# An opening program of its own for the first three chunks of a fused attention and two-expert kernel

## The chip, the cores and the metric

The kernel runs on one core of one Trainium2 chip. The metric is the device time of a whole execution in microseconds (us); lower is better. The kernel before took 826.4 us in the median of 3 runs (826.23 to 827.62).

The engines are named as in the profile: PE is TensorE (PEld its loading of weights), DVE is VectorE, ACT is ScalarE, POOL is GpSimd, SP is SyncE, which only issues transfers.

## The reference

```python
# attention with a decayed state: 4 batches, 8 heads, 768 tokens, 48 channels
for t in range(S):
    cur = einsum('bhd,bhe->bhde', u[None] * k[t], v[t])
    y[t] = einsum('bhd,bhde->bhe', r[t], state + cur)
    state = w[t][:, :, :, None] * state + einsum('bhd,bhe->bhde', k[t], v[t])
x = y.transpose(0, 2, 1, 3).reshape(3072, 384)
# first expert: 384 -> 1024 -> 384
h = x @ w_in
e = exp(h - max(h)); solu = h * e / (sum(e) + 1e-9)
ln = (solu - mean(solu)) / sqrt(var(solu) + 1e-6) * g_ln
x2 = ln @ w_out
# second expert: 384 -> 2048 -> 384
h2 = x2 @ w_in2
out = maximum(0.01 * h2, h2) @ w_out2
```

All arrays are float32.

## The kernel before, in words

**Tiles.** The 768 tokens of a batch are 6 chunks of 128 tokens. Three chunks are one super-tile of 384 tokens, so that there are 24 chunks and 8 super-tiles. Heads go in 4 pairs. TensorE has two ways to multiply: a float32 product, which the trace shows as two instructions, and an fp32r product of one instruction. Every large matrix product is made of three fp32r products: both operands are split into a high part (a copy that is rounded to fp32r) and a low part (the value less the high part), and high by high, low by high and high by low are added up. So each of the four weight matrices (W1 and W2 of the first expert, W3 and W4 of the second) stands in SBUF as `W1H`, `W1L` and so on. The raw load of a matrix lies where its low part will be (`W1raw` over `W1L`).

**A chunk is 8 items.** Item s=1 transposes the chunk's end keys (`transpose_keys`), s=2 to 5 make the scores of the 4 pairs (TensorE, masked by VectorE in `mask`), s=3 to 6 multiply the masked scores by the values and the queries by the state (`attend` in the changed kernel), s=6 also makes the fresh state, s=7 transposes y and splits it, and s=8 is the product by W1 (`expert_in`, 18 instructions with 512 columns). Softmax and layer norm of the 1024 hidden values follow in the next chunk's items: `row_max`, `exp_rows`, `times_exp`, `row_stats`, `row_moments`, `row_scale` (GpSimd), `normalise`. `prepare` makes the decays of the next chunk: four scans, four reciprocals, one product (VectorE), then `decayed_queries` and `end_keys` on GpSimd.

**A super-tile is 24 steps.** 8 steps M1 transpose the normalised rows (`prod`, three transposes), split them and multiply them by W2 (`cons`, nine instructions with 384 columns). 16 steps M2 multiply by W3 (`prod`, nine instructions), take the leaky maximum, split and multiply by W4 (`cons`, nine). `cons` runs two steps behind `prod`. Beside every step one item of a coming chunk is issued, on every engine in the order of the program text. The items lead by `LEAD` = 28: before the first M1 step items 1 to 28 are run alone (chunks 0 to 2, and half of chunk 3), and when the first M2 step begins 36 items are done.

**The weights.** ScalarE makes the high parts and VectorE or GpSimd the low parts, in 18 pieces of 1024 columns, tied to items by the table `when`. W2 is first multiplied by the layer norm's gain on GpSimd (L471). TensorE waits for all of W1's pieces before the first chunk's second half of columns, for W2's before the first M1 step and for W3's and W4's before the first M2 step (`wait_split`). SyncE loads chunk m+2's decays and chunk m+1's tokens when chunk m's buffers come free: there are two buffers of `att` and one of the tokens.

## Time and profile before

| | us |
|---|---|
| median of 3 runs | 826.4 |
| the profiled execution's own time | 825.48 |
| its span | 823.7 |
| first M2 product starts (from the span's start) | 114.25 |
| TensorE busy in the span | 786.2 (95%) |
| VectorE busy | 521.3 (63%) |
| GpSimd busy | 196.7 (24%) |

The page's slices cut the span into 40 parts of 20.6 us, each digit being the busy share in tenths. A row of a group gives line, engine, operation, output and inputs, shape and count, then busy time in us and mean ns of one, then the idle time of the engine ahead of it with what ended it. A time of the timeline is counted from the span's start; a row there can be several like instructions merged, and its duration holds the pipeline's delay, so that what an instruction costs is read from the start of one to the start of the next. The windows give the same busy times for stretches that one chooses.

### The profile page before, as it was taken

To read this page: it belongs to the slowest core of one execution; us is meant where nothing else is said; L and a number is where in the kernel's file an instruction comes from. 1 tells how busy PE (TensorE), PEld (TensorE's weight loads), DVE (VectorE), ACT (ScalarE), POOL (GpSimd) and SP (SyncE) were. 2 spreads that over 40 slices of the span, in tenths; PEclk is the share of its full clock that TensorE was granted. 3 is DMA by queue.
4 is the path that set the end of the run, shared out by engine and by line. 5 is a ranking of instruction groups with operands and counts; after the bars stand their busy time and mean duration, and the time that the engine had idled before them with its cause. 6 is when DMAs were issued, how large, how long until landed. Compare 5 with 4: busy or idle time off the path is not lost.

```text
span 823.7 us, 11957 instructions
## 1 busy us (share of the span) xinstructions
PE 786.2 (95%) x4570; PEld 746.2 (91%) x4570; DVE 521.3 (63%) x1068; ACT 338.8 (41%) x652; POOL 196.7 (24%) x216
## 2 busy tenths in 40 slices
PE   2877999999999999999999999999999999999996
PEld 2655999999999999999999999999999999999996
DVE  7778776576575676667665765666765775553332
ACT  3335644344433444434434444335443444334332
POOL 4477823113111221121221131122131121000000
PEclk9976899999999999999999999999999999999999
DMA  7772211203202302203202122113112030000000
GB/s 193 248 228 58 58 30 29 58 2 87 58 1 58 87 1 58 58 1 88 58 1 58 28 61 58 29 29 87 29 30 58 1 87 30 1 1 29 1 0 32
DMA packets 18847, 43.50 MB, mean 53 GB/s; under 512 B 2272, under 2 KB 14688, under 8 KB 18400
## 3 DMA queue, kind: packets, MB, share of 16 engines
q1 hardware_dynamic: 14736, 33.24, 16.5%
q10 hardware_dynamic: 4048, 9.44, 3.3%
q8 instruction: 37, 0.61, 0.3%
q14 instruction: 26, 0.21, 0.1%
HBM read 37.95 MB, written 4.72 MB: 52 GB/s over the span
## 4 chain that ended last, share of the span: by engine, by line
PE 85%; DVE 0%; ACT 0%; issue 0%; ACTq 0%
PE BANKS L964 60%; PE MISC L964 21%; PE BANKS L1075 2%; PE MISC L994 1%; PE MISC L987 1%; DVE Rraw L863 0%; DVE RL L869 0%; ACT RH L633 0%; ACT Rraw L626 0%; DVE X2L L875 0%; ACT X2H L638 0%; ACT OUT L644 0%; DVE A L745 0%; DVE nmean L817 0%; ACTq L248 0%
## 5 line engine op out<-in xcount | busy, mean ns | idle before, releaser
L626 ACT ACTIVATE Rraw<-BANKS 128x384 f32<-128x384 f32 x128 | 62.9, 492 | 239.5 <-PE BANKS L964 237.8
L863 DVE TENSOR_TENSOR Rraw<-BANKS,Rraw 128x384 f32<-128x384 f32 x128 | 71.3, 557 | 133.5 <-ACT Rraw L626 133.0
L964 PE MATMUL BANKS<-RH,W4H 128*128 128x384 f32 x384 | 138.6, 361 | 0.9 <-DVE RL L869 0.8
L964 PE MATMUL BANKS<-X2H,W3H 128*128 128x384 f32 x384 | 130.4, 339 | 0.2 <-DVE X2L L875 0.2
L964 PE MATMUL BANKS<-X2L,W3H 128*128 128x384 f32 x384 | 129.1, 336 | 0.0
L964 PE MATMUL BANKS<-RL,W4H 128*128 128x384 f32 x384 | 129.1, 336 | 0.0
L964 PE MATMUL BANKS<-X2H,W3L 128*128 128x384 f32 x384 | 129.0, 336 | 0.0
L964 PE MATMUL BANKS<-RH,W4L 128*128 128x384 f32 x384 | 129.0, 336 | 0.0
L633 ACT ACTIVATE RH<-Rraw 128x384 fp32r<-128x384 f32 x128 | 67.1, 524 | 73.2 <-DVE Rraw L863 73.2
L436 POOL TENSOR_TENSOR ke<-att 112x512 f32<-112x512 f32 x24 | 29.5, 1230 | 255.3 <-DVE att L739 255.3
L735 DVE RECIPROCAL ki<-att 112x128 f32<-112x128 f32 x96 | 90.1, 941 | 0.0
L869 DVE TENSOR_TENSOR RL<-Rraw,RH 128x384 fp32r<-128x384 f32 x128 | 72.5, 567 | 23.1 <-ACT RH L633 23.1
L460 POOL TENSOR_TENSOR rstd<-vare,mhalf 128x1 f32<-128x1 f32 x24 | 18.5, 771 | 245.2 <-DVE vare L818 245.2
L964 PE MATMUL MISC<-rb,att 112*128 112x256 f32 x192 | 61.3, 403 | 13.9 <-DVE att L739 13.3
L964 PEld LDWEIGHTS BANKS<-RH,W4H 128*128 128x128 f32 x384 | 72.3, 188 | 2.4 <-DVE RL L869 1.4
L964 PEld LDWEIGHTS BANKS<-RH,W4L 128*128 128x128 f32 x384 | 72.5, 189 | 1.0
L964 PEld LDWEIGHTS BANKS<-X2H,W3H 128*128 128x128 f32 x384 | 72.1, 188 | 0.5 <-issue 0.5
L964 PEld LDWEIGHTS BANKS<-X2H,W3L 128*128 128x128 f32 x384 | 72.1, 188 | 0.0
L964 PEld LDWEIGHTS BANKS<-RL,W4H 128*128 128x128 f32 x384 | 72.1, 188 | 0.0
L964 PEld LDWEIGHTS BANKS<-X2L,W3H 128*128 128x128 f32 x384 | 72.1, 188 | 0.0
L964 PE MATMUL BANKS<-RH,W2H 128*128 128x384 f32 x192 | 68.8, 358 | 0.0
L964 PE MATMUL BANKS<-RL,W2H 128*128 128x384 f32 x192 | 64.7, 337 | 0.0
(117 smaller groups left out, 1509.3 us busy)
## 6 DMA issues: line engine op xcount, KB each, us to landing
att<-rkw SPq DMA_DIRECT2D x48, 288.0 KB, 4.9
rtok<-r_tok SPq DMA_DIRECT2D x24, 192.0 KB, 4.5
ktok<-k_tok SPq DMA_DIRECT2D x24, 192.0 KB, 4.6
vtok<-v_tok SPq DMA_DIRECT2D x24, 192.0 KB, 4.7
out<-OUT SPq DMA_DIRECT2D x8, 576.0 KB, 5.6
W3raw<-w_in ACTq DMA_DIRECT2D x1, 3072.0 KB, 11.2
W4raw<-w_out ACTq DMA_DIRECT2D x1, 3072.0 KB, 24.3
W1raw<-w_in ACTq DMA_DIRECT2D x1, 1536.0 KB, 9.5
```

The lines of the kernel that those rows point to most:

```text
L436: nc.gpsimd.tensor_tensor(ke[:, :, :], kt[:, p, :, :], last, ALU.mult).then_inc(pool_ke, 1)
L460: nc.gpsimd.tensor_tensor(rstd[:, :], vare[:, :], mhalf[:, :], ALU.pow).then_inc(pool_rstd, 1)
L626: nc.scalar.activation(Rraw[:, fp % 2, :], PR[fp % 2][:, 0:ST], ACT.Copy, scale=0.01).then_inc(act_slope, 1)
L633: nc.scalar.activation(RH[:, fp % 2, :], src, ACT.Copy).then_inc(act_hi, 1)
L735: nc.vector.reciprocal(ki[:, a, :], ct[:, m % 2, a, :]).then_inc(dve_inv, 1)
L863: nc.vector.tensor_tensor(Rraw[:, fp % 2, :], PR[fp % 2][:, 0:ST], Rraw[:, fp % 2, :], ALU.max).then_inc(dve_relu, 1)
L869: nc.vector.tensor_tensor(RL[:, fp % 2, :], full, RH[:, fp % 2, :].bitcast(F32), ALU.subtract).then_inc(dve_lo, 1)
L964: return nc.tensor.matmul(dst, lhsT, rhs, start=start, stop=stop, skip_group_check=True)
L987: last = nc.tensor.transpose(XT[:, k * CH:(k + 1) * CH], rtok[:, k * 128:(k + 1) * 128], ident[:, :])
L994: last = nc.tensor.transpose(keys_of(b, m)[:, a * PD:(a + 1) * PD], ke[:, a, :], ident[0:PD, 0:PD])
L1075: last = nc.tensor.transpose(dst[:, c * CH:(c + 1) * CH], LN[:, c, f * 128:(f + 1) * 128], ident[:, :])
```

## The change

The first three chunks no longer go through items and M1 steps. They have an order of their own, written out for each engine.

- Decays, keys, queries and tokens of chunks 0, 1 and 2 have a buffer each (`att2`, `tok12`, `A2` lie in the space of W4's high part, which is filled later), and SyncE issues all their loads at the start. ScalarE issues the loads of W1, W3 and W2 one behind the other.
- For these chunks both products of the first expert are float32 products on the raw weights: `first_expert` is 6 products with 512 columns (two instructions each) in place of 18 fp32r ones, and `first_out` is 24 products with 128 columns for each chunk. y and the normalised rows are not split. The rows are transposed by `first_rows` and multiplied by the gain on the way out of PSUM (`take_ln`, 8 ACTIVATEs of 128 columns).
- W1 and W2 are split later, in the first M2 steps, and W2's gain is no longer multiplied in by GpSimd; later M1 steps multiply by it when they take the rows from PSUM (ScalarE and VectorE, `step` and `step_lo`).
- All low parts are made by GpSimd (`low_part`), in 24 groups of 768 columns: W3's eight and W4's first while the opening runs, the other 15 in the 16 steps of the first M2 stage.
- The opening ends with 24 items done (chunks 0 to 2). The first M2 stage has 28 items in its 16 steps in place of 16, so that from the first M1 step on the items stand as before.
- In the opening the scans read their floor from PSUM (`FLOOR_PS`), masks are made for two pairs at once, and the first chunk's keys in two halves.
- TensorE multiplies the identity by itself eight times, unread, before the first scores.

```diff
+        if opening and fp <= STEPS:
+            done = [CPS * SLOTS + (F1 + LEAD - CPS * SLOTS + F2) * j // F2 for j in (f, f + 1)]
+        else:
+            done = [fp + LEAD - 1, fp + LEAD]
+        listed.append((k, so, f, fp, [slot_of(i) for i in range(done[0] + 1, done[1] + 1)]))
...
+        att2 = sb("att2", [PD, 3, PAIRS, CH], over="W4H", skip=3 * F2 * MODEL // 8 * 4)
+        A2 = sb("A2", [CH, PAIRS, 2, CH], over="W4H")
...
+        tok12 = [sb(f"tok{m}", [CH, 3, MODEL], over="W4H", skip=(5 * F2 // 8 + 3 * (m - 1)) * MODEL * 4) for m in (1, 2)]
...
+        FLOOR_PS = PR[1][0:PD, 511:512]
...
-        when = {0: 3, 1: 5, 2: 7, 3: 15, 4: 16, 5: 17, 6: 18, 7: 20, 8: 21, 9: 23, 10: 23, 11: 23,
-                12: 27, 13: 28, 14: 29, 15: 30, 16: 31, 17: 32}
-        by_dve = (0, 1, 2, 3, 4, 9, 10, 11)
...
+        GROUPS = (4, 4, 8, 8)
...
-            load_T(0, 1)
-            for i in range(1, LEAD + 1):
-                item(0, *slot_of(i))
-            for kind, so, f, fp, m, s in first_steps():
-                item(0, m, s)
+            for m in (1, 2):
+                load_T(0, m)
+                load_tok(0, m)
+            load_tok(0, 3)
+            load_T(0, 4)
+            load_T(0, 3)
...
+            def low_part(w, g):
+                pool.wait_ge(split_hi[w], g + 1)
+                if w == 0:
+                    pool.wait_ge(pe_h, 2 * CPS)
+                if w == 1:
+                    pool.wait_ge(pe_cons, F1)
+                nc.gpsimd.tensor_tensor(group(los[w], w, g), group(raws[w], w, g),
+                                        group(his[w], w, g).bitcast(F32), ALU.subtract).then_inc(split_lo[w], 1)
...
+                    if opening(b, kind, so):
+                        if f % 2 == 0 and f // 2 + 1 < GROUPS[3]:
+                            low_part(3, f // 2 + 1)
+                        if f < GROUPS[0]:
+                            low_part(0, f)
+                        if F1 <= f < F1 + GROUPS[1]:
+                            low_part(1, f - F1)
...
+            decayed_queries(0, 2)
+            decayed_state(0, 1)
+            own_token(0, 1, 1)
+            own_token(0, 2, 0)
+            end_keys(0, 2)
+            decayed_state(0, 2)
+            own_token(0, 2, 1)
+            row_scale(0, 0)
+            for g in range(2):
+                low_part(2, g)
+            row_scale(0, 1)
+            for g in range(2, 4):
+                low_part(2, g)
+            row_scale(0, 2)
+            decayed_queries(0, 3)
+            for g in range(4, 6):
+                low_part(2, g)
+            end_keys(0, 3)
+            for g in range(6, 8):
+                low_part(2, g)
+            low_part(3, 0)
...
+            take_keys(0, 0)
+            part_heads(0, 1)
+            take_x(0, 0)
+            take_range(0, 1)
+            take_keys(0, 1)
+            part_heads(0, 2)
+            take_range(0, 2)
+            take_x(0, 1)
+            take_keys(0, 2)
+            load_weights(3)
+            exp_rows(0, 0)
+            for g in range(2):
+                high_part(2, g)
+            take_x(0, 2)
+            normalise(0, 0)
+            exp_rows(0, 1)
+            take_ln(0)
+            normalise(0, 1)
+            exp_rows(0, 2)
+            for g in range(2, 4):
+                high_part(2, g)
+            take_ln(1)
+            normalise(0, 2)
+            for g in range(4, 6):
+                high_part(2, g)
+            part_heads(0, 3)
+            for g in range(6, 8):
+                high_part(2, g)
+            take_ln(2)
+            take_range(0, 3)
+            for g in range(2):
+                high_part(3, g)
+            take_x2(0, 0)
+            for g in range(4):
+                high_part(0, g)
...
+                    nc.scalar.activation(RH[:, fp % 2, :], PR[fp % 2][:, 0:ST], ACT.Identity,
+                                         scale=gain[:, f:f + 1]).then_inc(act_hi, 1)
...
+            decay(0, 1)
+            first_mask(0, 0)
+            own_sums(0, 0)
+            first_mask(0, 2)
+            for a in (0, 1):
+                inverse(0, 1, a)
+            take_y(0, 0)
+            take_state(0, 0)
+            for a in (2, 3):
+                inverse(0, 1, a)
+            undecayed_keys(0, 1)
+            decay(0, 2)
+            for a in (0, 1):
+                inverse(0, 2, a)
+            for a in (0, 2):
+                first_mask(1, a)
+            own_sums(0, 1)
+            for a in (2, 3):
+                inverse(0, 2, a)
+            undecayed_keys(0, 2)
+            take_y(0, 1)
+            take_state(0, 1)
+            for a in (0, 2):
+                first_mask(2, a)
+            own_sums(0, 2)
+            row_max(0, 0)
+            take_y(0, 2)
+            take_state(0, 2)
+            times_exp(0, 0)
+            row_stats(0, 0)
+            row_moments(0, 0)
+            row_max(0, 1)
+            times_exp(0, 1)
+            row_stats(0, 1)
+            row_moments(0, 1)
+            row_max(0, 2)
+            times_exp(0, 2)
+            row_stats(0, 2)
+            row_moments(0, 2)
+            decay(0, 3)
+            for a in range(PAIRS):
+                inverse(0, 3, a)
+            undecayed_keys(0, 3)
+            take_x2(0, 0)
...
+            def first_expert(m, halves=(0, 1)):
+
+                pe.wait_ge(act_x, m + 1)
+                if m == 0:
+                    pe.wait_ge(ld_w[0], 16)
+                if m == 1:
+                    pe.wait_ge(dve_masked, CPS * PAIRS)
+                for n in halves:
+                    for k in range(KM):
+                        last = mm(hidden(0, m)[:, n * 512:(n + 1) * 512], X[:, k, :], w1[:, k, n * 512:(n + 1) * 512],
+                                  k == 0, k == KM - 1)
+                    last.then_inc(pe_h, 1)
...
+            def first_rows(m):
+
+                pe.wait_ge(act_ln, m + 1)
+                if m == 0:
+                    pe.wait_ge(dve_decay, CPS * PAIRS)
+                    pe.wait_ge(dve_state, CPS)
+                if m == 1:
+                    pe.wait_ge(dve_he, 4)
+                for f in range(F1):
+                    if m == 2 and f % 4 == 0:
+                        pe.wait_ge(act_lnT, F1 + f + 4)
+                    last = nc.tensor.transpose(ln_bank(m, f // 4)[:, f % 4 * CH:(f % 4 + 1) * CH],
+                                               LN[:, m, f * 128:(f + 1) * 128], ident[:, :])
+                    if f % 4 == 3:
+                        last.then_inc(pe_lnT, 1)
...
+            def first_out(m):
+
+                if m == 0:
+                    pe.wait_ge(dve_he, 4)
+                    pe.wait_ge(ld_w[1], 16)
+                for f in range(F1):
+                    pe.wait_ge(act_lnT, m * F1 + f + 1)
+                    for k in range(KM):
+                        last = mm(ACC[k][:, m * CH:(m + 1) * CH], w2[:, f, k * 128:(k + 1) * 128], first_ln[:, f, :],
+                                  m == 0 and f == 0, f == F1 - 1)
...
+            for _ in range(8):
+                mm(ACC[0][:, 0:128], ident[:, :], ident[:, :], True, True)
+            first_scores(0, range(PAIRS))
+            first_attend(0, (0, 1))
+            first_keys(0)
+            first_attend(0, (2, 3))
+            first_state(0)
+            first_transposes(0)
+            first_expert(0, (0,))
+            first_scores(1, range(PAIRS))
+            first_keys(1)
+            first_attend(1, range(PAIRS))
+            first_state(1)
+            first_scores(2, range(PAIRS))
+            first_expert(0, (1,))
+            first_transposes(1)
+            first_keys(2)
+            first_attend(2, range(PAIRS))
+            first_state(2)
+            first_expert(1)
+            first_transposes(2)
+            first_rows(0)
+            first_expert(2)
+            first_out(0)
+            for m in (1, 2):
+                first_rows(m)
+                first_out(m)
             for b in range(B - 1):
-                run(b, batch_steps(False))
+                run(b, batch_steps(False, b == 0))
```

The order on TensorE at the start of the first M2 stage, before (`RH`, `RL` are split rows, `X2H`, `X2L` the split input of the second expert, `rb` and `att` the operands of scores, `A` the masked scores, `vtok` the values):

```order
238 L964 MATMUL BANKS<-RH,W2L 128x384
239 L964 MATMUL BANKS<-RL,W2H 128x384
240 L964 MATMUL MISC<-rb,att 128x256 [waits dve_masked,split_lo2,split_lo]
241 L964 MATMUL MISC<-state,att 128x96 [waits dve_masked]
242 L964 MATMUL MISC<-vtok,A 128x48 x2
243 L964 MATMUL BANKS<-X2H,W3H 128x384 [waits dve_x2,dve_lo]
```

The same place after (`OUT` holds the transposed rows, `W2raw` the raw weights, `ke` the end keys):

```order
110 L1122 MATMUL BANKS<-OUT,W2raw 128x128 [waits act_lnT]
111 L1122 MATMUL BANKS<-OUT,W2raw 128x128 x2
112 L1122 MATMUL BANKS<-OUT,W2raw 128x128 [waits act_lnT]
113 L1122 MATMUL BANKS<-OUT,W2raw 128x128 x2
114 L1146 MATMUL MISC<-ident,ke 128x112 [waits pool_ke,dve_state]
115 L1146 MATMUL MISC<-ident,ke 128x112 x3
116 L1122 MATMUL BANKS<-X2H,W3H 128x384 [waits dve_x2,split_lo2]
```

The item ahead of the first M2 product is now item 25 (chunk 3, s=1) and was item 37 (chunk 4, s=5).

The order on GpSimd from the second chunk's queries to the end of the opening, after (`tok_84` are chunk 2's tokens, `att_74` its decays, queries and keys; `W3L` is a low part):

```order
37 L502 TENSOR_TENSOR tok_84<-tok_84,diag 128x384 [waits dve_diag]
38 L510 TENSOR_TENSOR rstd<-vare,mhalf 128x1 [waits dve_var]
39 L512 TENSOR_TENSOR nbias<-nmean,rstd 128x1 [waits pool_rstd]
40 L520 TENSOR_TENSOR W3L<-W3raw,W3H 128x3x256 [waits split_hi2] x2
41 L510 TENSOR_TENSOR rstd<-vare,mhalf 128x1 [waits act_ln,dve_var]
42 L512 TENSOR_TENSOR nbias<-nmean,rstd 128x1 [waits pool_rstd]
43 L520 TENSOR_TENSOR W3L<-W3raw,W3H 128x3x256 [waits split_hi2] x2
44 L510 TENSOR_TENSOR rstd<-vare,mhalf 128x1 [waits act_ln,dve_var]
```

Low parts of W3 now stand between the row scales of the three chunks, where the queue of before had pieces of W2 and W3.

## Rows read from the trace of the kernel before

**Rows 1.** The page: busy time, then TensorE and its granted clock in 40 slices.

```profile
PE 786.2 (95%) x4570; PEld 746.2 (91%) x4570; DVE 521.3 (63%) x1068; ACT 338.8 (41%) x652; POOL 196.7 (24%) x216
...
PE   2877999999999999999999999999999999999996
...
PEclk9976899999999999999999999999999999999999
```

**Rows 2.** Windows, all engines: stretch, length, busy by engine (instructions), granted clock, DMA.

```profile
27.00:113.23 86.23, 71.97 (x332) 60.84 (x332) 66.01 (x128) 41.38 (x66) 61.70 (x50) 0.80 0.44 128
113.23:182.47 69.24, 69.23 (x411) 66.65 (x410) 44.99 (x95) 28.25 (x57) 12.31 (x14) 1.00 0.14 35
182.47:207.73 25.26, 25.26 (x155) 23.89 (x156) 17.31 (x37) 11.78 (x24) 6.63 (x8) 1.00 0.27 71
```

**Rows 3.** The chain that ended last: start, us, what (merged).

```profile
117.67 1.43 PE MISC L964 x14
...
124.14 4.19 PE MISC L964 x18
...
765.13 47.95 PE BANKS L964 x270
```

**Rows 4.** Timeline of TensorE: start, duration, instruction, count.

```profile
27.58 0.63 PE L964 MATMUL BANKS<-W1L,XH 128*128 128x512 f32 x1
...
28.01 0.63 PE L964 MATMUL BANKS<-W1H,XL 128*128 128x512 f32 x1
...
92.42 0.49 PE L1075 MATMUL BANKS<-ident,LN 128*128 128x128 f32 x3
92.70 0.50 PE L964 MATMUL MISC<-W1H,XH 128*128 128x512 f32 x1
...
113.23 0.60 PE L964 MATMUL MISC<-rb,att 112*128 112x256 f32 x2
113.66 0.35 PE L964 MATMUL MISC<-state,att 112*128 112x96 f32 x2
113.86 0.57 PE L964 MATMUL MISC<-vtok,A 128*128 128x48 f32 x4
114.25 0.42 PE L964 MATMUL BANKS<-X2H,W3H 128*128 128x384 f32 x1
```

**Rows 5.** Windows, TensorE alone: stretch, length, busy, granted clock, DMA.

```profile
28.00:29.00 1.00, 1.00 (x4) 1.00 0.85 154
...
57.00:66.00 9.00, 8.94 (x39) 0.50 0.00 0
90.00:91.00 1.00, 1.00 (x8) 0.76 0.00 0
```

**Rows 6.** Timelines of VectorE and GpSimd, in this order.

```profile
7.84 1.37 DVE L727 TENSOR_TENSOR_SCAN att<-att,floor 112x128 f32<-112x128 f32 x4 [3.56 <-DMA att<-rkw]
...
13.81 3.28 DVE L727 TENSOR_TENSOR_SCAN att<-att,floor 112x128 f32<-112x128 f32 x4 [0.59 <-DMA att<-rkw]
...
92.56 3.13 DVE L739 TENSOR_TENSOR att<-att,ki 112x512 f32<-112x512 f32 x1
...
88.06 7.08 POOL L477 TENSOR_TENSOR W4L<-W4raw,W4H 128x1024 fp32r<-128x1024 f32 x3
```

**Rows 7.** Groups by form: VectorE (first two), ScalarE (two), GpSimd (one).

```profile
L735 DVE RECIPROCAL ki<-att 112x128 f32<-112x128 f32 x96 | 90.1, 941 | 0.0
...
L798 DVE TENSOR_TENSOR LN<-MISC,LN 128x512 f32<-128x512 f32 x28 | 18.0, 687 | 7.5 <-ACT LN L560 7.5
...
L567 ACT ACTIVATE LN<-EXP,nbias,rstd 128x1024 f32<-128x1024 f32 x8 | 9.9, 1243 | 3.9 <-POOL nbias L462 3.5
...
L555 ACT ACTIVATE W4H<-W4raw 128x1024 fp32r<-128x1024 f32 x6 | 6.2, 1048 | 0.0
...
L428 POOL TENSOR_TENSOR att<-att 112x508 f32<-112x508 f32 x24 | 30.7, 1281 | 7.1 <-DVE att L727 7.1
```

**Rows 8.** DMA issues of the first 60 us: size, median us to landing.

```profile
ub<-u SPq DMA_DIRECT2D x1, 192.0 KB, 6.2
```

More of the change, by code:

```diff
@@ L61, in slot_of, with batch_steps @@
     return (item - 1) // SLOTS, (item - 1) % SLOTS + 1
-def batch_steps(last):
+def batch_steps(last, opening=False):
     out = []
@@ L1008, in item @@
                 p = m % 2
-                if first(b, m) and 1 <= m and 1 <= s <= 3:
-                    expert_in(b, m - 1, s - 1, 3)
-                if s == 1 and not first(b, m):
+                if s == 1:
                     if m % CPB > 0:
```

541 lines of the change are left out of this document (291 added, 250 removed).

## The prediction

> **What bounds the kernel now.** I read the page first. TensorE is busy 95% of the span, and all that is missing lies in the first five slices and the last; the granted clock is below full only there too [rows 1]. The windows then cut the start by stage [rows 2]. From 113.23 us on TensorE has no gap: 69.23 of 69.24 us in the first M2 stage, 25.26 of 25.26 in the next M1 stage. From 27 to 113.23 it is busy 71.97 of 86.23 us at a mean clock of 0.80. So behind the first M2 product, which starts at 114.25 [rows 4], the kernel costs what TensorE has to do, and ahead of it what chains between engines and the low clock allow. The end is the start of that product plus a fixed remainder, 823.7 - 114.25 = 709.45 us. The change earns what it brings that start forward, and pays for the items that it then has still to run.
>
> **Prices on TensorE at full clock.** Starts in a row give them [rows 4]: a pair's scores 0.43 us (two instructions of 256 columns), its state product 0.20, its values 0.39 (four instructions of 48 columns), three transposes 0.28. An fp32r `expert_in` is 4.19 us, and the 14 instructions of item 6 are 1.43, so the fresh state is 1.43 - 0.59 = 0.84 [rows 3]. A float32 product has two instructions of 0.215 us per 256 columns. That makes 0.86 us for 512 columns and 5.2 us for a `first_expert`, and 0.215 us for 128 columns, 5.2 us for a `first_out`. At low clock both double, as 512 columns of fp32r do: 0.43 us from start to start at 28 us [rows 4], and 4.19/18 = 0.23 at full clock [rows 3]. The granted clock of that window reads 1.00 [rows 5], so before the first change of clock I go by the spacing, which is 1.2 GHz.
>
> **The opening, step by step.** DVE: first scans 1.37 us [rows 6], a reciprocal 0.94 (0.84 from start to start), a product of 512 columns 0.69 [rows 7], and I take a maximum or a statistics instruction of that width alike. ACT: normalise 1.24, high parts of 768 columns 1.05 x 0.75 = 0.8 [rows 7], the exponent, as wide as the normalise, 1.3; an ACTIVATE of 128 columns 0.27 by estimate, an eighth of 1.05 and as much again for its start. POOL: queries 1.28 [rows 7], low parts 7.08/3 x 0.75 = 1.8 [rows 6].
> - Chunk 0. The decays land at about 7.4 (0.4 earlier, fewer memsets ahead of the load). POOL now waits for `ub` before its first queries: `ub` took 6.2 us to land [rows 8], which is about 10.8. First scores follow at 12.4, behind ScalarE's copies. The scores at low clock take 3.4 us, masks, values, keys and fresh state run to 22.2, y is transposed by 23.1 and the first expert starts at 23.8 (before: 27). The eight products of the identity run from about 5 to 8.4 us, where TensorE has nothing else; cost 0.
> - First half of expert 0 at low clock 5.1 us, to 28.9. Scores of chunk 1 (keys ready at 25.4) follow, then masks and values, state, scores of chunk 2 at 35, the second half of expert 0 to 39.4, values of chunk 2 from 40.2 to 43.8.
> - Expert 1 from 43.8: the small products ahead of it leave the clock low. Of its 5.2 us some 2.3 double: to 51.5. y of chunk 2 at 52; ACT takes it (0.5) and only then normalises chunk 0 (1.24): rows at 53.7, TensorE waits 1.8 us. Transposes 0.8, expert 2 5.2: 59.7. Out 0: 65. Rows and out 1: 71.1. Rows 2 at 71.9. ACT has in its order by then one normalise, 6 high parts and the queries of chunk 3, 1.24 + 4.8 + 1.3 behind 66+2.2, so that `take_ln(2)` starts at about 73.8; out 2 to 79.4, X2 split, first M2 product at 81. Before: 114.25.
>
> From both sides: with no wait after 23.8 and full clock, three experts and three outs (31 us), two chunks' attention and the rest (14 us) end at 69. With the low clock for all that is not expert or out, and 4 us more of waits, at 89. I take 81, from the chain.
>
> **What it pays.** 12 items are moved behind that point: chunk 3 without its first and chunk 4's s=1 to 5. A whole chunk by these prices is 4.19 + 0.28 + 0.4 + 4 x (0.43 + 0.59) + 0.84 = 9.8 us, by the windows (69.24 - 16 x 18 x 47.95/270)/2 = 9.05 [rows 2, 3]; I take 9.5. Chunk 3 less its keys' transposes is 9.1, chunk 4's five 0.4 + 4 x 0.43 + 3 x 0.59 = 3.9: together 13.0 us.
>
> The first M2 stage becomes 69.2 + 13 = 82.3 us for TensorE. VectorE had 44.99 us in it with two chunks of items [rows 2]; 16 steps are about 18 of these, so a chunk is 13.5 and 3.5 chunks 47: 65 of 82. POOL gets 3.5 x 6.2 + 15 x 1.8 = 49. Cover is there, but items now stand two to a step. From the end of an expert to the scores that may overwrite its sums, maximum, exponent and product need 0.7 + 0.2 + 1.3 + 1.3 + hops, 4.1 us, and TensorE has about 3.6 us of work between them, where it had two whole steps: some 1 to 1.5 us lost for each of three chunks. ScalarE also does four high parts of W1 (3.2 us) ahead of the first M2 step, about 1 us. I take 5 us; the ends are 0 and 14. The gain moved into M1's copies costs nothing: VectorE is busy 17.31 of 25.26 us there and TensorE has no gap [rows 2], and GpSimd is rid of its eight products. The loads carry the bytes of before and stand earlier in their queues. Two matrices and two chunks more are now in flight at once, but W1 is wanted at 23.8 and chunk 1's tokens at 31; I take 0, and if the tokens came a few us late it would lie in the 89 above, no further.
>
> The last item is the port. The product of keys took 3.13 us, where one of the same width takes 0.69 [rows 7], while POOL made three low parts in a row [rows 6]; scans took 3.28 instead of 1.37 once. The floor in PSUM should end it for scans. It stays for keys and for every split of W4's input, whose operands are both in SBUF, against 15 low parts: bounded by 0 and 15 x 1.8 = 27 less VectorE's 17 us of slack, 10; it is in the 14 above. The Trainium skill's page "SBUF — State Buffer", section "SBUF: two separate sides", calls the pair of ports that VectorE and GpSimd share an exclusive lock, held for the whole instruction, for a VectorE instruction with two SBUF inputs. The trace agrees with it in the 3.13 us.
>
> **Sum.** 709.45 + 81 + 13 + 5 = 808.5 us span. What lies around it was 825.48 - 823.7 = 1.8 us: 810.3, and the profiled execution was 0.9 under the median of 826.4. So 811 us, 15.4 less, 1.9%. Its own range runs from the bounds together (start at 69 with 2 us of stalls, 89 with 10) to 796 and 824; the ends seldom meet, and 801 to 819 holds most of it.
>
> **Rivals.**
> 1. The clock stays low in the outs (slower). The outs are products of 128 columns with weights loaded for each, like the attention's small ones, through which TensorE was 99% busy from 57 to 66 us at a granted clock of 0.50 [rows 5]. Then three outs cost 15.6 us more, first M2 product at 97, and with 3 us of stalls in the chain between, 827 span and 830 us. Against it: experts of 512 columns stand ahead, under which the clock always rose, and it rose at 90 us [rows 5] under small products too. It decides from a start of 97 on. Chance 0.08.
> 2. The port is the bound. All 24 low parts hold VectorE up by most of their 1.8 us: 14 us in the opening, of which 7 come through, and 10 in the stage, of which 5 are already counted: 811 + 12 = 823 us, still faster by 0.4%. For it: rows 6. Against it: most of VectorE's operands are in PSUM. Chance 0.13.
> 3. The opening is quicker than my chain: clock full from 28 us on, ScalarE's late work hidden, start at 73 and 3 us of stalls: 801 us. For it: TensorE's own work ends at 69. Against it: in the opening before no engine was ever free of the others. Chance 0.21.
>
> **Chances.** Forecast 0.58, the rest as above. What a measurement can tell from no change here is 0.2%, 1.7 us. Faster 0.91, within 0.2% 0.03, slower 0.06. Range 798 to 820: it leaves out rival 1, most of rival 2 and the fastest of rival 3.
>
> **What would show it.** First M2 product at 76 to 86 us (before 114.25). TensorE about 13 us more in the first M2 stage, which is 85 to 90 us long, with gaps ahead of scores with s=2. From the next M1 stage on stages of 25.3 and 69.4 us as before. A granted clock of 1.00 through the outs; first rows' transposes waiting for `LN`. Wrong would be: outs spaced at 0.43 us, VectorE's product of keys or splits at 2 us in the stage's windows, or a start beyond 95.

## The result, and the profile after

The changed kernel takes 833.36 us in the median of 4 runs (833.14 to 833.72), the kernel before 826.32 (825.82 to 827.62) beside it: 0.8% slower, ratio 1.0083 [1.0066, 1.0101]. The forecast was 811 us, and the time lies outside the range. The profiled execution has a span of 831.7 us, 8.0 more than before.

The page of the profile after answers to [rows 1]. First the busy time, then the 40 slices:

```profile
PE 790.4 (95%) x4640; PEld 743.9 (89%) x4640; DVE 513.2 (62%) x1044; ACT 344.9 (41%) x676; POOL 207.9 (25%) x226
...
PE   5998888789999999999999999999999999999996
...
PEclk9999999899999999999999999999999999999999
```

The head of the kernel is filled, but the holes of slices 5 to 9 lie where [rows 1] had nines. The windows of the profile after (stretch, length, busy by engine with instructions, granted clock, DMA) answer to [rows 2]: the opening, the first M2 stage, the first M1 stage, then the second M1 and the third M2 stage. (The prediction cut its windows at other places, 69.24 and 25.26 us long; their lengths are not to be set against these.)

```profile
0.00:77.44 77.44, 64.82 (x358) 50.60 (x358) 49.70 (x97) 37.19 (x81) 42.86 (x52) 1.00 0.65 194
77.44:182.21 104.77, 86.44 (x472) 79.00 (x472) 69.10 (x131) 43.72 (x81) 51.40 (x43) 0.95 0.14 34
182.21:213.63 31.42, 30.92 (x183) 29.17 (x184) 20.20 (x42) 13.00 (x25) 6.61 (x8) 0.95 0.21 58
279.75:309.97 30.22, 29.76 (x189) 28.07 (x187) 21.23 (x44) 13.99 (x27) 6.62 (x8) 1.00 0.22 59
309.97:374.87 64.90, 64.90 (x383) 62.71 (x383) 41.76 (x88) 26.34 (x52) 12.31 (x14) 1.00 0.16 37
```

The first M2 stage and the second M1 stage of the kernel before, cut in the same way at the first product of each:

```profile
114.25:179.19 64.94, 64.94 (x382) 62.75 (x382) 41.76 (x88) 26.33 (x52) 12.31 (x14) 1.00 0.15 37
...
274.67:304.32 29.65, 29.65 (x189) 28.12 (x187) 20.78 (x44) 13.50 (x27) 6.61 (x8) 1.00 0.24 61
```

So the first M2 product comes 36.8 us earlier (114.25 to 77.44). The first M2 stage then takes 104.77 us in place of 64.94, which is 39.8 more. The first M1 stage takes 31.42 in place of 29.37 (2.05 more), and the six behind it together 3.5 us more. Later M2 stages are the same but for 0.3 us in all. With 0.9 us less behind the last stage's first product that makes 8.0 us. The whole gain of the opening is spent in one stage, where TensorE has nothing to do for 18.3 of 104.77 us.

The gaps that come of it are many. TensorE's first instruction behind each of the longer ones (in brackets the gap and what ended it):

```profile
84.07 0.57 PE L1122 MATMUL MISC<-state,att 112*128 112x96 f32 x2 [2.06 <-issue]
95.03 0.46 PE L1122 MATMUL MISC<-state,att 112*128 112x96 f32 x2 [1.57 <-DVE A L847]
101.28 0.50 PE L1122 MATMUL MISC<-W1H,XH 128*128 128x512 f32 x1 [1.07 <-DVE XL L893]
114.78 0.43 PE L1122 MATMUL MISC<-state,att 112*128 112x96 f32 x2 [1.47 <-issue]
...
139.58 0.67 PE L1122 MATMUL MISC<-rb,att 112*128 112x256 f32 x2 [1.18 <-DVE LN L910]
145.88 0.46 PE L1122 MATMUL MISC<-state,att 112*128 112x96 f32 x2 [0.97 <-DVE A L847]
...
176.95 0.62 PE L1122 MATMUL MISC<-vtok,A 128*128 128x48 f32 x4 [1.18 <-DVE A L847]
182.21 0.52 PE L1301 MATMUL BANKS<-ident,LN 128*128 128x128 f32 x3 [2.20 <-ACT LN L636]
```

The largest is 5.27 us. The timelines of TensorE, VectorE and GpSimd in the profile after, 147 to 157 us (start, duration, instruction, and in brackets the idle time ahead with what ended it):

```profile
150.71 0.33 PE L1122 MATMUL BANKS<-X2L,W3H 128*128 128x384 f32 x1
156.32 0.74 PE L1122 MATMUL MISC<-state,att 112*128 112x96 f32 x2 [5.27 <-DVE A L847]
```

```profile
149.48 0.94 DVE L836 RECIPROCAL ki<-att 112x128 f32<-112x128 f32 x1
150.34 5.59 DVE L981 TENSOR_TENSOR RL<-Rraw,RH 128x384 fp32r<-128x384 f32 x1
155.85 0.41 DVE L847 TENSOR_TENSOR A<-MISC,causal 128x256 f32<-128x256 f32 x1
```

```profile
147.58 1.83 POOL L520 TENSOR_TENSOR W4L<-W4raw,W4H 128x768 fp32r<-128x768 f32 x1
149.37 1.83 POOL L520 TENSOR_TENSOR W2L<-W2raw,W2H 128x768 fp32r<-128x768 f32 x1
151.18 0.82 POOL L502 TENSOR_TENSOR rtok<-vtok,diag 128x384 f32<-128x384 f32 x1
151.96 1.79 POOL L520 TENSOR_TENSOR W2L<-W2raw,W2H 128x768 fp32r<-128x768 f32 x1
153.72 1.79 POOL L520 TENSOR_TENSOR W4L<-W4raw,W4H 128x768 fp32r<-128x768 f32 x1
```

Followed back: TensorE waits for the mask of a step's second item. The mask itself takes 0.41 us, but stands on VectorE behind the split `RL`, two operands in SBUF, which usually takes 0.49 to 0.56 us and here takes 5.59. It ends at 155.93, when GpSimd has come through its row of five instructions (155.5). Behind the gap TensorE is slow too; the windows of TensorE alone:

```profile
151.00:156.30 5.30, 0.05 (x1) 0.96 0.00 0
156.30:163.00 6.70, 6.68 (x23) 0.52 0.38 89
163.00:170.00 7.00, 7.00 (x37) 1.00 0.28 84
```

After 5.3 us with nothing to do it works at the lower level (0.52, which is about 1.2 of 2.4 GHz) until 163. 6.7 us at 0.52 are 3.2 us lost, on top of the 5.3.

### The profile page after: what moved, and what is told of

The parts are those of the page before. It is cut to its first block, busy times and chain, and to the rows that moved or that the text cites. A ratio compares the mean times of both kernels' runs of the same rounds, so it can differ in the third digit from the quotient of the medians.

```text
span 831.7 us, 12171 instructions
## 1 busy us (share of the span) xinstructions
PE 790.4 (95%) x4640; PEld 743.9 (89%) x4640; DVE 513.2 (62%) x1044; ACT 344.9 (41%) x676; POOL 207.9 (25%) x226
## 4 chain that ended last, share of the span: by engine, by line
PE 76%; DVE 3%; ACT 2%; issue 1%; ACTq 0%
PE BANKS L1122 53%; PE MISC L1122 20%; PE BANKS L1301 2%; DVE EXP L910 1%; PE MISC L1139 1%; ACT EXP L629 1%; PE MISC L1146 1%; DVE hmax L900 1%; DVE RL L983 0%; DVE RL L981 0%; ACT RH L703 0%; DVE Rraw L974 0%; ACT Rraw L697 0%; ACT RH L701 0%; DVE nmax L903 0%
## 5 line engine op out<-in xcount | busy, mean ns | idle before, releaser
L1122 PE MATMUL BANKS<-X2H,W3H 128*128 128x384 f32 x384 | 132.3, 344 | 0.7 <-DVE X2L L989 0.7
L981 DVE TENSOR_TENSOR RL<-Rraw,RH 128x384 fp32r<-128x384 f32 x128 | 80.5, 629 | 23.6 <-ACT RH L701 23.6
L510 POOL TENSOR_TENSOR rstd<-vare,mhalf 128x1 f32<-128x1 f32 x24 | 13.2, 550 | 251.9 <-DVE vare L930 251.9
L900 DVE TENSOR_REDUCE hmax<-MISC 128x1 f32<-128x512 f32 x44 | 30.4, 691 | 57.0 <-PE MISC L1122 57.0
L1122 PE MATMUL MISC<-rb,att 112*128 112x256 f32 x176 | 54.8, 396 | 6.7 <-DVE EXP L910 2.9
L1122 PE MATMUL BANKS<-RH,W2H 128*128 128x384 f32 x168 | 60.8, 362 | 0.0
```

Of the source, the lines that this page charges most:

```text
L510: nc.gpsimd.tensor_tensor(rstd[:, :], vare[:, :], mhalf[:, :], ALU.pow).then_inc(pool_rstd, 1)
L900: nc.vector.reduce_max(hmax[:, n:n + 1], hidden(b, m)[:, n * 512:(n + 1) * 512], AX.X).then_inc(dve_max, 1)
L981: nc.vector.tensor_tensor(RL[:, fp % 2, :], Rraw[:, fp % 2, :], hi, ALU.subtract).then_inc(dve_lo, 1)
L1122: return nc.tensor.matmul(dst, lhsT, rhs, start=start, stop=stop, skip_group_check=True)
```

## The experiments

All are the changed kernel with one edit, unless said. Ratios are to the kernel before, whose median beside them was 825.5 to 826.5 us. "Stage" is the first M2 stage, from its first product to the first transposes of M1.

**e1: GpSimd's low parts made thin.**

```diff
-        w1r = [t[:, :].rearrange("p (k n) -> p k n", k=KM) for t in (W1H, W1L)]
+        w1r = [t[:, :].rearrange("p (k n) -> p k n", k=KM) for t in (W1H, W1H)]
...
-                            low_part(0, f)
+                            low_part(0, f, 8)
```

W2 and W4 have the same two edits; the 8 is the number of columns.

> This kernel leaves out most of the low parts of W1, W2 and W4: GpSimd's 16 subtractions for them are 8 columns wide, and TensorE multiplies by the high parts a second time where it multiplied by the low ones, so it has the same products. All else is the changed kernel (833.4 us, first M2 stage 104.8 us long with 18.3 us of idle TensorE). If GpSimd's low parts hold up VectorE's split RL and so the mask and TensorE, the 5.28 us gap at 151 and the 1.6 us gap at 93 go, and the clock's loss behind them, about 84 to 88 and 156 to 163: 6.5 us of gaps and some 5 us of clock, so 820 to 824 us, stage 93 to 96 us. If instead two items in a step are simply too long a chain for VectorE (scans, moments and statistics ahead of the mask), nearly all of the idle time stays: 830 to 834 us, stage over 100 us.

Measured: 820.58 us, ratio 0.9948 [0.9923, 0.9973], 12.8 us under the changed kernel and in the range of the first theory. The seven runs go from 819.25 to 824.50 us, three of them at 824.1 or more; the trace is of a run of 819.53 us (span 817.4, 14.3 less), and what follows is read from it. Its stage:

```profile
76.28:168.49 92.21, 82.12 (x471) 74.57 (x472) 60.70 (x131) 43.61 (x81) 26.54 (x41) 1.00 0.16 39
```

GpSimd is busy 24.9 us less, and VectorE, whose instructions are the same 131, 8.4 us less: so much of its busy time was waiting. The idle time falls from 18.3 to 10.1 us and the clock stays at 1.00 throughout. So 12.6 us of the stage come from the 15 low parts that GpSimd makes in it. The next M1 stage has 29.86 us in place of 31.42, and both begin behind the same wait for `LN` of 2.20 us, in the changed kernel with a fall of the clock and here without. These 1.6 us are not shown to be the low parts': e10 has all of them, the same wait, a clock of 1.00 and 29.9 us.

**e2: GpSimd lets the split pass first.**

```diff
                     if opening(b, kind, so):
+                        pool.wait_ge(dve_lo, marks(b, fp))
```

> One part is added to the changed kernel: in the first M2 stage GpSimd starts the low parts of a step only when VectorE has done that step's split RL. If the low parts of several steps in a row are what kept RL at 5.59 us beside them, the 5.28 us gap at 151 shrinks to under 1.5 us, the clock does not drop behind it, and the time is 822 to 827 us. If the low parts only move and meet the mask or the next split instead, the stage stays within 3 us of 104.8 and the time is 830 to 835 us.

Measured: 832.53 us, 1.0083 [1.0066, 1.01]; stage 103.1. The large gap went (1.81 us in its place), and two others came. TensorE in e2, then VectorE ahead of the first of these gaps:

```profile
88.59 0.74 PE L1123 MATMUL MISC<-state,att 112*128 112x96 f32 x2 [3.73 <-DVE A L848]
104.42 0.47 PE L1123 MATMUL MISC<-W1H,XH 128*128 128x512 f32 x1 [2.60 <-POOL W1L L520]
```

```profile
82.55 5.20 DVE L829 TENSOR_TENSOR_SCAN att<-att,floor 112x128 f32<-112x128 f32 x4
```

The low parts now met the scans, which took 5.20 us for four in place of 1.36, ahead of a mask; and W1's last low part came too late for the first `expert_in` of the stage. The second theory of the text held (830 to 835): moving them does not make the contention less.

**e3: ScalarE's high parts of W1 moved into the steps.** W2's four high parts move too, from steps 1, 3, 5 and 7 to steps 4 to 7.

```diff
-            for g in range(4):
-                high_part(0, g)
...
+                        if f < GROUPS[0]:
+                            high_part(0, f)
```

> ScalarE's four high parts of W1 go from ahead of the first step into the steps 0 to 3 of the first M2 stage, one each, and W2's four into steps 4 to 7. If they hold the first steps (ScalarE's 3.06 us ahead of the first mask and the 2.06 us gap at 82), the gap at 82 goes and with it the lower clock up to 88: 2 to 4 us, so 829 to 832 us. If the gap at 82 is VectorE's own, or a high part delays the relu copies by as much in later steps, the time is 833 us or above, up to 836.

Measured: 840.81 us, 1.0178 [1.0161, 1.0195], slower than either theory allowed; stage 111.7. What I had left out is the chain behind a high part:

```profile
103.16 1.80 POOL L520 TENSOR_TENSOR W1L<-W1raw,W1H 128x768 fp32r<-128x768 f32 x1 [5.91 <-ACT W1H L625]
```

W1's last low part begins at 103.2 and `expert_in` waits 4.42 us for it, and the gap at 82 turned into one of 3.03 at 87.6. W1's high parts at the stage's start were well placed; what W2's four added is not told apart.

**e4: no gain in M1.** The kernel leaves the multiplication by the gain out.

```diff
-                    nc.scalar.activation(RH[:, fp % 2, :], PR[fp % 2][:, 0:ST], ACT.Identity,
-                                         scale=gain[:, f:f + 1]).then_inc(act_hi, 1)
+                    nc.scalar.activation(RH[:, fp % 2, :], PR[fp % 2][:, 0:ST], ACT.Copy).then_inc(act_hi, 1)
...
-                    nc.vector.scalar_tensor_tensor(RL[:, fp % 2, :], PR[fp % 2][:, 0:ST], gain[:, f:f + 1], hi,
-                                                   ALU.mult, ALU.subtract).then_inc(dve_lo, 1)
+                    nc.vector.tensor_tensor(RL[:, fp % 2, :], PR[fp % 2][:, 0:ST], hi, ALU.subtract).then_inc(dve_lo, 1)
```

> This kernel leaves the scale (gain) out in M1 of every super-tile: ScalarE copies PR and VectorE subtracts, without the multiplication. If the multiplication is what made each M1 stage 0.6 us longer than before (six stages, and part of the first), the M1 stages are back at 29.1 and 29.65 us and the time is 3.5 to 4.5 us less, 829 to 830 us. If their length is set by something else (the wait of TensorE at the stage's two ends), it stays at 833.

Measured: 833.13 us, 1.008 [1.0063, 1.0097]. The M1 stages have 30.07 and 29.67 us in place of 30.25 and 29.87: 0.2 us each where the text asked for 0.6. Their main cost was something else. The rows by form, changed kernel and then e4:

```profile
L703 ACT ACTIVATE RH<-BANKS,gain 128x384 fp32r<-128x384 f32 x56 | 32.5, 580 | 67.0 <-PE BANKS L1122 66.4
```

```profile
L703 ACT ACTIVATE RH<-BANKS 128x384 fp32r<-128x384 f32 x56 | 27.5, 490 | 69.4 <-PE BANKS L1120 68.8
```

**e5: one wait as before the change.** Compared instruction by instruction, the M1 stages of both kernels start each instruction within 0.01 us of the other up to 17.3 us into the stage; there the changed kernel has this gap:

```profile
296.73 0.49 PE L1301 MATMUL BANKS<-ident,LN 128*128 128x128 f32 x3
297.68 0.67 PE L1122 MATMUL MISC<-rb,att 112*128 112x256 f32 x2 [0.46 <-DVE EXP L910]
```

The first scores of a chunk overwrite the second half of the last chunk's hidden values, which VectorE multiplies first; before, they waited for that product alone, now for both.

```diff
-                        wait(pe, dve_he, chunks(b, m, 2))
+                        wait(pe, dve_he, chunks(b, m, 2, -1))
...
                     if a == 0:
+                        wait(pe, dve_he, chunks(b, m, 2))
                         wait_tok(pe, b, m)
```

> One wait is put back as it was before the change: TensorE's first scores of a chunk wait for the first of VectorE's two products with EXP (which frees their bank of MISC), and its first output product waits for the second; in the changed kernel the scores wait for both. If that wait is what makes each M1 stage 0.57 us longer (TensorE idle 0.46 us behind VectorE's EXP product at 17.9 us into the stage), the six later M1 stages are back at 29.65 and 29.1 us, the first stages gain up to 1 us, and the time is 829 to 830 us. If the M1 stages stay at 30.2 us, it is something else, and the time 833 us.

Measured: 831.58 us, 1.0061 [1.0044, 1.0077]. The five full M1 stages behind the first have 29.83 and 29.37 us: 0.45 each, 2.2 in all. Its stage is 0.4 longer (105.2) and the M1 stage behind it 0.9, so 1.8 us came through. e4 and e5 together are what M1 lost, as e12 shows.

**e6: VectorE makes the low parts itself.** GpSimd's `low_part` calls of the stage, and the one for W4's first piece, are taken out; the same calls stand at the end of VectorE's steps, with

```diff
+                nc.vector.tensor_tensor(group(los[w], w, g), group(raws[w], w, g),
+                                        group(his[w], w, g).bitcast(F32), ALU.subtract).then_inc(split_lo[w], 1)
```

> The 16 low parts of W1, W2 and W4 that GpSimd computed beside the first M2 stage are computed by VectorE, at the end of the same steps. If the trouble is that GpSimd's and VectorE's two-input work wait for one another (the port theory), the split RL is back at 0.49 us, the 5.28 us gap goes, and VectorE's 16 times about 0.85 us fit into its idle time between the steps: 820 to 825 us, first M2 stage 92 to 96 us. If the trouble is the amount of work ahead of the mask on VectorE, whoever does it, the added 13.6 us on VectorE make it worse or no better: 832 to 840 us.

Measured: 830.05 us, 1.0043 [1.0027, 1.006]; stage 101.3, between the two theories. `RL` is at its normal length (564 ns in the mean, 629 in the changed kernel) and the 5.27 us gap is gone. But at the end of a step a low part stands ahead of the next mask, and its fourth piece of W1 made `expert_in` wait 2.63 us.

**e7: masks ahead of statistics.** VectorE issues `item()` of a step's second item ahead of `item_end()` of its first.

> VectorE issues the mask (and the take of the outputs) of a step's second item ahead of the first item's statistics and moments. If the order inside a step of two items costs the gaps of 2.06, 1.47, 1.18 and 0.97 us that end with a mask, half of them go: 2 to 3 us less, 830 to 831.5 us. If the masks wait for TensorE's own products or for RL behind GpSimd, nothing changes: 833 us, and the 5.28 us gap stays in both cases.

Measured: 834.38 us, 1.0093 [1.0073, 1.0112]; stage 104.7. Two gaps ahead of a second item's product went (1.57 and 0.97) and one shrank from 1.47 to 0.31, but another grew from 0.83 to 1.15, one of 0.58 came, and the large one grew to 6.77. In all TensorE is idle 1.6 us less, and the stage is no shorter for it. No gain while the large one stands.

**e8: the twelve items alone.**

```diff
+            for i in range(CPS * SLOTS + 1, F1 + LEAD + 1):
+                item(0, *slot_of(i))
```

This stands on every engine ahead of the first M2 step, with `item_mid`, `item_end` and `prepare` where an engine has them; W1's four low parts go there too.

> The twelve items 25 to 36 run alone ahead of the first M2 stage instead of beside it, in pairs; the stage has 16 items again as before the change, and only the low parts of W4 and W2 stay in it. By theory 2 (two items in a step are what costs) the stage is back at 65 to 67 us, and the twelve items alone, a chain of about 3 us each without cover, lengthen the opening by 30 to 38 us: 826 to 835 us. By the port theory alone the stage keeps a part of its idle time, since 12 low parts stay beside it, and is 70 us or longer, and the time is 835 us or more.

Measured: 828.04 us, 1.0025 [1.0012, 1.0038]. The windows of its opening's second part and its stage:

```profile
80.00:110.60 30.60, 25.06 (x92) 20.27 (x92) 19.70 (x41) 6.45 (x12) 17.22 (x17) 0.61 0.18 39
110.60:178.10 67.50, 66.83 (x381) 64.36 (x382) 46.38 (x86) 33.47 (x62) 31.73 (x25) 0.98 0.14 36
```

With one item a step the stage is 67.5 us with 0.67 of idle TensorE, though W4's and W2's low parts are in it and GpSimd is busy 31.7 us. VectorE was held up there as well:

```profile
145.36 4.12 DVE L989 TENSOR_TENSOR RL<-Rraw,RH 128x384 fp32r<-128x384 f32 x1
```

So the low parts alone do not open gaps: it takes two items in a step as well, whose second mask stands right behind `RL`. The price moved: alone the twelve items lengthen the opening by some 33 us, most of it at a granted clock near 0.5.

**e9: W2's low parts in the last four steps.**

```diff
-                        if F1 <= f < F1 + GROUPS[1]:
-                            low_part(1, f - F1)
+                        if F2 - GROUPS[1] <= f:
+                            low_part(1, f - (F2 - GROUPS[1]))
```

> GpSimd's four low parts of W2 stand in the last four steps (12 to 15) of the first M2 stage instead of steps 8 to 11, so they no longer follow W4's back to back at 148 to 155; nothing else changes. By the port theory (a split RL that finds GpSimd busy with one low part after another waits until the row of them ends) the 5.27 us gap at 151 goes, and the clock's fall behind it: 6 to 9 us less, 824 to 828 us. If that gap is from the two items' own work on VectorE at that step, it stays, and the time is 832 to 835 us.

Measured: 833.57 us, 1.0084 [1.0065, 1.0102], a miss. The gap shrank to 3.47 us but did not go. (The gap of 1.57 us ahead of 95.03 is 3.17 here, and 3.17 in e10 as well, so it differs between executions.) VectorE, then GpSimd:

```profile
149.19 3.80 DVE L981 TENSOR_TENSOR RL<-Rraw,RH 128x384 fp32r<-128x384 f32 x1
```

```profile
149.00 1.81 POOL L520 TENSOR_TENSOR W4L<-W4raw,W4H 128x768 fp32r<-128x768 f32 x1
150.78 1.79 POOL L520 TENSOR_TENSOR W2L<-W2raw,W2H 128x768 fp32r<-128x768 f32 x1
```

GpSimd runs ahead of TensorE: it waits for nothing in these steps, so that pieces of several steps still follow each other. `RL` again ends with the last of the row (152.6). What was gained there came back in the M1 stage behind, 33.6 us long.

**e10: without the identity products.**

> The eight unread products of the identity are taken out. If they warm TensorE's clock for the first scores, the opening gets 0.5 to 2 us longer: 834 to 835.5 us. If they do nothing (their end at 10.1, the first scores at 12.4, both still in the low clock), nothing changes within 0.3%: 833 us, and the span may even be shorter, since it begins with the first instruction recorded.

Measured: 833.74 us, 1.0082 [1.0059, 1.0104], no change. First scores at 12.08 (12.42 with them), both at the low spacing. Its stage has 105.1 us and the M1 stage behind it 29.9.

**e11: e6 in better places.** The low part comes between the step's first mask and its relu product; W1's in steps 0, 0, 2 and 3, W2's in 12 to 15.

> VectorE computes the 16 low parts as in e6, but between a step's first mask and its relu product, where it mostly waits for TensorE, and W1's four earlier (two in step 0) and W2's in the last four steps. In e6 two gaps were the low parts' own place: 3.11 us at 85 (mask behind W4L and W1L) and 2.63 us at 103.6 (the expert waits for W1L). If they go: 4 to 7 us less than e6, 823 to 826 us. If VectorE's amount of work (about 75 us of the stage) is the bound and not its order, it stays at 829 to 831 us.

Measured: 824.93 us, 0.9977 [0.9965, 0.9989]; stage 94.9, within 3 us of e1's, though all the work of the low parts is done. It is 6.4 us shorter than e6's, whose VectorE does the same work: order mattered, not amount. The M1 stage behind it takes 32.8 us, 3.0 more than e1's; e14 deals with this.

**e12: e11, e5's wait, and the gain multiplied into W2 at its split.**

```diff
+                        last = nc.scalar.activation(W2H[:, cols], W2raw[:, cols], ACT.Identity, scale=gain[:, f:f + 1])
...
+                        last = nc.vector.scalar_tensor_tensor(W2L[:, cols], W2raw[:, cols], gain[:, f:f + 1],
+                                                              W2H[:, cols].bitcast(F32), ALU.mult, ALU.subtract)
```

> e11, and with it the scores' wait for the first product with EXP alone (as in e5, 1.8 us less), and the gain multiplied into W2's high and low parts when they are split, so that M1's copies have none (as in e4, 0.2 us in each of seven M1 stages). If the three add up: 3 us less than e11, so 820 to 823 us, faster than before the change (826.4). If VectorE's place in the first stage loses what e5 gained there (its stage was 0.4 us longer), 822 to 825 us.

Measured: 822.76 us, 0.9947 [0.9931, 0.9964]. Later M1 stages have 29.53 and 29.10 us (before: 29.65 and 29.10): the 0.45 and the 0.2 are all of M1's loss.

**e13: e12 with the twelve items alone.**

> e12's edits (low parts on VectorE, one product with EXP waited for, gain in W2's split) with the twelve items 25 to 36 alone ahead of the stage, as in e8. e8 had no idle TensorE in its stage, which took 67.5 us, and the first M2 product at 110.6. If the edits save there what they save elsewhere (about 3.9 us in the M1 stages, 1 to 2.5 us in the stage), 822 to 824 us, the same as e12: two items beside a step and twelve alone would then cost alike. If the twelve items alone also get shorter without GpSimd's low parts beside them, 818 to 821 us. If VectorE's low parts lengthen the chain of items alone, 825 us or more.

Measured: 828.45 us, 1.0049 [1.0026, 1.0073], no better than e8: first M2 product at 112.6, and from 76 to 112 us a granted clock of 0.63. Beside the steps the same items are 5.7 us cheaper (e12).

**e14: e12 with W2's low parts in steps 5, 7, 9 and 11.**

> e12 with VectorE's four low parts of W2 in steps 5, 7, 9 and 11 instead of 12 to 15. In e12 the last of them took 2.14 us at 168 beside GpSimd and held the relu product, ScalarE's RH and then LN, so that TensorE waited 2.84 us at the end of the stage (172.4) with the clock at 0.50 up to 179. If that is the cause of the wait, it shrinks to 2 us or less and the stage and the next are 1.5 to 4 us shorter: 819 to 821.5 us. If the wait comes from the last chunk's own statistics, which are due then in any case, it stays, and the time is 822 to 823.5 us.

Measured: 819.82 us, 0.9929 [0.9913, 0.9946]. The wait for `LN` before M1 fell from 2.84 to 2.19 us, the two stages from 127.8 to 126.0.

**e15: e14 with the items spread in another way,** two to a step in steps 0 to 11, one in 12 to 15.

```diff
-            done = [CPS * SLOTS + (F1 + LEAD - CPS * SLOTS + F2) * j // F2 for j in (f, f + 1)]
+            done = [CPS * SLOTS + min(2 * j, F1 + LEAD - CPS * SLOTS + j) for j in (f, f + 1)]
```

> e14 with the 28 items of the first M2 stage given to its steps in another way: two in each of the steps 0 to 11 and one in each of 12 to 15. If the gap ahead of M1 and the low clock after it come from the pile of work in the last steps, they go: 2 to 4 us less than e14. If the early steps, which are already short of work for VectorE's masks (gaps of 1.6, 0.8 and 1.1 us), lose more than that, it is slower than e14 by 1 to 4 us. The same within 1 us would mean that the idle time only moves with the items.

Measured: 814.93 us, 0.9881 [0.9862, 0.9901], the fastest, 18.4 us under the changed kernel and 1.2% under the kernel before. Its stage and the M1 stage behind it:

```profile
76.10:168.97 92.87, 83.45 (x471) 76.20 (x472) 75.56 (x148) 44.28 (x83) 24.77 (x27) 0.98 0.17 39
168.97:198.20 29.23, 29.23 (x186) 27.68 (x184) 20.38 (x43) 13.53 (x27) 6.63 (x8) 1.00 0.22 62
```

The last steps are light, `LN` is ready when M1 begins (no gap there, 2.19 in e14), and the M1 stage is at full clock. VectorE is busy 75.56 us, more than in the changed kernel (69.10), and the stage is 11.9 us shorter.

## Why the prediction was wrong

**The opening was right.** First M2 product at 77.44, predicted 81, bounds 69 and 89 (76.0 to 78.0 in the runs whose opening is the same). Steps of the chain in the profile after:

```profile
6.33 3.78 PE L1122 MATMUL BANKS<-ident 128*128 128x128 f32 x16 [6.33 <-POOL heads L573]
12.42 4.17 PE L1122 MATMUL MISC<-rb,att 112*128 112x256 f32 x8 [2.31 <-ACT rb L646]
...
23.54 5.49 PE L1122 MATMUL BANKS<-W1raw,X 128*128 128x512 f32 x6 [0.58 <-ACT X L653]
...
43.47 5.34 PE L1122 MATMUL BANKS<-W1raw,X 128*128 128x512 f32 x12
...
50.84 0.65 PE L1265 MATMUL BANKS<-ident,LN 128*128 128x128 f32 x4 [1.71 <-ACT LN L636]
...
51.77 5.32 PE L1122 MATMUL MISC<-W1raw,X 128*128 128x512 f32 x12
...
71.02 5.60 PE L1122 MATMUL BANKS<-OUT,W2raw 128*128 128x128 f32 x48 [1.12 <-ACT OUT L711]
```

First scores were predicted at 12.4 and came at 12.42, the first expert 23.8 and 23.54, the wait for the normalised rows 1.8 and 1.71. The 3.6 us gained are mostly expert 1 (the row at 43.47), done in 5.2 us from start to start where the chain had 7.7: "the small products ahead of it leave the clock low" did not hold. The first condition of rival 3 did hold: products are at full spacing from about 30 us on. Rival 1 fell with the last row: the 48 instructions of a `first_out` take 5.43 us from start to start, 0.113 us each, and the price at full clock was 0.108. The 7 us that rival 2 had come through in the opening did not come. The identity products were 0, as said (e10).

**The moved items were right in TensorE's work.** Counting e1's stage against before's at before's prices from start to start gives 16 more scores at 0.215, 18 expert instructions at 0.233, 28 values at 0.098, 14 state products at 0.10 and 1.5 us of transposes and fresh state: 13.3 us, predicted 13.0. TensorE's busy time rose by 17.2 (82.12 less 64.94), so 3.9 us are left, by inference instructions drawn out beside short waits, which the profile counts as busy.

**The step that failed is "I take 5 us; the ends are 0 and 14", the term for waits in the first M2 stage.** Measured in the stage: 18.3 us idle, those 3.9, and 4.3 us of low clock (86.44 less 82.12), so 26.5 against 5, and 1.6 more of low clock in the M1 stage. The prediction's own sign of being wrong, splits at 2 us, is there too: 5.59. By cause:
- Of it 12.6 us go with GpSimd's low parts (e1). The port was known and half of rival 2 was this, but its bound subtracted VectorE's 17 us of slack from 27 us of low parts. Slack at other times does not pay for a wait: one split held 5.59 us, with TensorE's next instruction behind it. And what such a gap costs does not end with it: clock, 4.3 of 12.6 us in the stage. The prediction priced no clock in the stage at all. The row from which it took its rule of the port, 3.13 us for the product of keys, cannot bear it out: the product started at 92.56, just where one of three low parts gave way to the next (88.06 and two thirds of 7.08 make 92.78), and so does not tell whether it waited for one instruction or through two.
- The other 14, 10.1 us idle in e1 and those 3.9, go with two items in a step: with one item there is 0.67 us of idle TensorE (e8). The prediction named scores behind an expert, three times 1 to 1.5 us; the gap of 1.18 us that EXP's product (`LN` L910) ended is one of these, but the masks behind scans, statistics and moments, `XL` ahead of the expert and `LN` ahead of M1 were not counted. The place of each instruction decides: e11 gives the low parts to VectorE, the busier engine, and its stage is 9.9 us shorter; e15 only shifts items, and its stage is 2.4 us shorter than e14's. How the 14 divide among these waits is not shown.
- The 1.6 us of clock in the M1 stage stand behind the wait for `LN`; e1 and e10 have the wait and not the fall.
- The high parts of W1 were called about 1 us. Moving them, with W2's, made it worse by 7 us (e3), which does not price them where they stood.

**"The gain moved into M1's copies costs nothing" failed too,** by 0.2 us a stage: 580 ns for 490 on ScalarE (e4), in the chain from a stage's first rows to their products. And the wait for both products with EXP, 0.45 us in each M1 stage (e5), was in the new text of `item` and I had not seen it. Together 3.5 us over six stages. That TensorE has no gap before is no proof that nothing lies within a few tenths of it.

With 26.5 and 1.6 in place of 5, and 3.5 in place of 0, less the 3.6 of the opening, the prediction's sum is 811 + 21.5 + 1.6 + 3.5 - 3.6 = 834 us, against 833.4 measured.

What stays open: why three of e1's seven runs are 4 to 5 us longer than the other four, how the 9.4 us of idle TensorE left in e15's stage divide among its gaps' causes, and why `RL` waits through a row of GpSimd's instructions in one place and only through one in another. The wait of e3's and e2's scans beside low parts was seen and not tried apart.

## What to carry to other kernels

When work is moved from a serial opening into a full stage, its busy time says little: look at what stands right behind each instruction that can wait, and at what TensorE has queued until then. Slack of an engine summed over a stage covers nothing at a given moment; put side work where the engine waits anyway, ahead of an instruction that itself waits for TensorE, and leave the last steps before a stage's end light. After rewriting a function compare each wait's count with the old one: a count that is larger by one cost 0.45 us in every full M1 stage.

## What the runs showed of the hardware

- A VectorE instruction with two operands in SBUF can wait through a whole row of GpSimd instructions: 5.59 us behind four of them, 3.80 behind two (e9), where alone it takes 0.49 to 0.56. Four scans took 5.20 us beside two low parts and two products for the tokens (e2; 1.36 alone). It does not always wait for the whole row: the split of the row below, from the profile after, went ahead once the low part that ended at 94.22 was done, though GpSimd had another in its row, which ran to 96.3. The Trainium skill's page "SBUF — State Buffer", section "SBUF: two separate sides", has the one that starts first hold the pair of ports for its whole instruction; by it `RL` would, by an estimate from these rows, have waited for the piece of W2 that began at 149.37, to 151.2, 0.9 us. The trace has 5.59, and the measurement decides: VectorE was not let in between two instructions of GpSimd there. The split at 92.75 agrees with the page.

```profile
92.75 1.89 DVE L981 TENSOR_TENSOR RL<-Rraw,RH 128x384 fp32r<-128x384 f32 x1
```

- The same subtraction of 768 columns takes 1.8 us on GpSimd and, where nothing holds it up, 0.81 to 0.87 from start to start on VectorE (e6). Three others in e6 lasted 1.79 to 2.02 us.
- The granted clock fell to 0.52 behind the gap of 5.27 us. In the same trace it fell for a shorter time behind the gaps of 2.06 and 2.20 us (windows of TensorE alone):

```profile
84.00:88.00 4.00, 3.93 (x16) 0.57 0.00 0
182.00:187.00 5.00, 4.79 (x23) 0.66 0.01 3
```

It did not fall behind gaps of 1.1 to 2.2 us in e1, nor behind the one of 2.20 in e10. So the length of a gap of about 2 us does not tell whether the clock falls.
- In the changed kernel's first 77.44 us the granted clock reads 1.00, but the eight instructions of chunk 0's scores take 4.04 us from start to start (12.42 to 16.46) and those of chunk 2 take 1.80 (34.92 to 36.72). The record of e1 reads 0.50 from 16 to 27 us, where TensorE does the same at the same spacing. Where the record reads full from the start, only the spacing tells.
